# Zeroing the scratch tensors of an attention + MLP + expert kernel from SBUF instead of from a DRAM constant

## The reference, cut to what matters

```python
# 1. attention in a window of 128 with a linear bias, 8 heads of 64 channels
scores = scale * q @ k.T + bias, masked;  attn = softmax(scores);  x = attn @ v
# 2. a dense MLP, 512 -> 2048 -> 512
r = np.maximum(x @ w_in, 0.0);  x = (s * (r * r) + b) @ w_out
# 3. experts: each token goes to the best 2 of 8, with noisy logits
noisy_logits = x @ w_gate + np.log1p(np.exp(x @ w_noise)) * noise
top2 = np.argpartition(-noisy_logits, 2, axis=1)[:, :2]     # weights: softmax over the two
for e in range(8):
    for k in range(2):
        mask = top2[:, k] == e
        h = np.maximum(x[mask] @ w1[e], 0.0)                 # 512 -> 1024
        out[mask] += top2_w[mask, k, None] * (h @ w2[e])     # 1024 -> 512
```

## Time and profile before

| what | value |
|---|---|
| median of 3 runs | 1090.13 us (1089.6 to 1093.48) |
| the profiled execution's own time | 1090.13 us |
| its span in the profile | 1088.3 us |
| PE busy | 1044.8 us, 96% |
| DVE, ACT, POOL busy | 60%, 44%, 11% |
| mean granted TensorE clock | 0.987 of full speed |
| bytes moved by DMA | 147.04 MB, mean 135 GB/s |

### The profile page before, as it was taken

How to read it: one execution, slowest core, us unless ns; L and a number is a source line. 1 busy time by engine, 2 the same in 40 slices (tenths; PEclk the granted TensorE clock), 3 DMA queues, 4 the chain that set the end, 5 groups by cost and what they waited for, 6 DMA issues and landing times.

```text
span 1088.3 us, 18159 instructions
## 1 busy us (share of the span) xinstructions
PE 1044.8 (96%) x5846; PEld 917.1 (84%) x5847; DVE 656.6 (60%) x1955; ACT 479.1 (44%) x988; POOL 117.9 (11%) x122
## 2 busy tenths in 40 slices
PE   5689999999999999999999999999999999999995
PEld 4588889889889888988989888888888889888884
DVE  6777866766776686664567845654545435445322
ACT  6756665555556456443445333333323323233211
POOL 0000000110020020010020111211121111211211
PEclk9799999999999999999999999999999999999998
DMA  6556754454463343122364525352523515423312
GB/s 185 151 176 202 229 160 153 160 175 145 155 214 102 93 146 98 49 72 104 97 223 155 178 79 175 96 185 72 172 90 112 180 61 185 137 83 101 129 30 97
DMA packets 76473, 147.04 MB, mean 135 GB/s; under 512 B 12012, under 2 KB 12652, under 8 KB 76272
## 3 DMA queue, kind: packets, MB, share of 16 engines
q1 hardware_dynamic: 67440, 125.91, 36.8%
q0 software_dynamic: 8960, 20.21, 5.3%
HBM read 125.09 MB, written 46.78 MB: 158 GB/s over the span
## 4 chain that ended last, share of the span: by engine, by line
PE 89%; DVE 4%; ACT 3%; issue 2%; DMA 1%; SPq 0%; DVEq 0%; POOL 0%; ACTq 0%; POOLq 0%
PE bank L1300 23%; PE bank L1302 23%; PE bank L1301 23%; PE bank L1441 8%; PE bank L1281 3%; PE bank L1268 2%; PE bank L1326 1%; PE bank L1247 1%; PE bank L1449 1%; PE bank L1248 1%; PE bank L1387 1%; PE bank L1394 1%; DVE x_sc L837 1%; ACT x_sc L610 1%; ACT w_now_hi L664 1%
## 5 line engine op out<-in xcount | busy, mean ns | idle before, releaser
L1300 PE MATMUL bank<-w_hi,g_hi 128*128 128x512 f32 x312 | 127.5, 409 | 1.2 <-DVE g_lo L1182 1.2
L1302 PE MATMUL bank<-w_hi,g_lo 128*128 128x512 f32 x312 | 122.4, 392 | 0.0
L670 ACT ACTIVATE relu<-bank 128x384 f32<-128x384 f32 x96 | 47.1, 491 | 170.7 <-PE bank L1302 170.5
L1301 PE MATMUL bank<-w_lo,g_hi 128*128 128x512 f32 x312 | 121.9, 391 | 0.0
L892 DVE SCALAR_TENSOR_TENSOR relu<-relu,sb_scale 128x384 f32<-128x384 f32 x96 | 59.3, 618 | 70.5 <-ACT relu L670 70.5
L532 POOL DMA_INDIRECT rows_scratch<-x,slot x36 | 39.2, 1090 | 522.6 <-DVE x L973 513.4
L759 ACT ACTIVATE g_hi<-bank 128x384 fp32r<-128x384 f32 x56 | 27.5, 492 | 141.4 <-PE bank L1302 141.4
L610 ACT ACTIVATE x_sc<-x_sc,least 128x256 f32<-128x256 f32 (+1 forms) x144 | 69.9, 488 | 12.2 <-DVE least L837 11.9
L1149 DVE SCALAR_TENSOR_TENSOR g_lo<-bank,g_hi 128x384 fp32r<-128x384 f32 x56 | 31.1, 556 | 72.6 <-ACT g_hi L759 72.4
L886 DVE TENSOR_TENSOR w_now_lo<-stage_a,w_now_hi 128x1024 fp32r<-128x1024 f32 x48 | 58.7, 1223 | 23.0 <-ACT w_now_hi L664 22.8
L837 DVE CUSTOM_DVE_ANT_0 x_sc<-bank,nbias 128x256 f32<-128x256 f32 (+1 forms) x144 | 52.9, 405 | 30.9 <-PE bank L1248 22.5
(11 more groups left out here) (210 smaller groups left out, 2751.1 us busy)
## 6 DMA issues: line engine op xcount, KB each, us to landing
stage_a<-in_w_first SPq DMA_DIRECT2D x92, 256.0 KB, 2.9
stage_a<-in_w_second SPq DMA_DIRECT2D x92, 256.0 KB, 3.1
qk_raw<-in_qk SPq DMA_DIRECT2D x144, 128.0 KB, 2.7
y_scratch<-in_blank SPq DMA_DIRECT2D x13, 768.0 KB, 5.9
stage_b<-in_w_first SPq DMA_DIRECT2D x28, 256.0 KB, 2.9
stage_b<-in_w_second SPq DMA_DIRECT2D x28, 256.0 KB, 3.8
rows_scratch<-in_blank SPq DMA_DIRECT2D x8, 774.0 KB, 6.5
rows<-rows_scratch SPq DMA_DIRECT2D x8, 774.0 KB, 7.1
```

The lines of the kernel that those rows point to most:

```text
L670: act.activation(relu[:, (t * C1 + c) % GR, :], h_bank[c % 2][:, 0:TOK1], ACT.Relu).then_inc(relu_ready, 1)
L1300: pe.matmul(psum, lh, rh, start=(first and n == 0), stop=False)
L1301: pe.matmul(psum, lh, rl, start=False, stop=False)
L1302: done = pe.matmul(psum, ll, rh, start=False, stop=(last and n == len(pairs) - 1))
```

## The change

The constant `blank` is gone. In the head POOL clears the tile `x2` once (128 partitions x 1548 floats), then puts 2^20 in the last column of the tile's first block (`zeroed`). SP waits for that after the head, and then fills both scratch tensors from `x2`, all of it in stage 0. `rows_dram` takes 24 DMAs of 128 rows (258 KB each), three in each of the slots 2 to 9. `y_dram` takes 13 DMAs of 384 rows (768 KB each), one in each of the slots 2 to 14. Since the first `copy_out` overwrites `x2`, ACT and DVE wait there until all 37 have landed (`zero_out`). The waits for `rows_blank` on POOL and `y_blank` on SP go.

```diff
+        zeroed = sem("zeroed")
+        zero_out = sem("zero_out")
+        ZEROS = (E * BLK2 + YROWS // TOK2) * 16
...
+                sp.wait_ge(zeroed, 1)
...
-                        if t == 0 and c % 2 and 3 <= c < 3 + 2 * E:
-                            at_ = (c - 3) // 2 * N
-                            sp.dma_start(rows_dram[at_:at_ + TOK2, :], a["blank"]).then_inc(rows_blank, 16)
-                        if 1 <= t and c % 2 and 3 <= c < 15:
-                            r = ((t - 1) * 6 + (c - 3) // 2) * TOK2
-                            if r < YROWS:
-                                sp.dma_start(y_dram[r:r + TOK2, :], a["blank"][:, 0:DM]).then_inc(y_blank, 16)
+                        if t == 0 and 2 <= c < 2 + E:
+                            for r in range(BLK2):
+                                at_ = (c - 2) * N + r * P
+                                sp.dma_start(rows_dram[at_:at_ + P, :], x2[:, 0, :]).then_inc(zero_out, 16)
+                        if t == 0 and c >= 2:
+                            for r in range((c - 2) * TOK2, min((c - 1) * TOK2, YROWS), TOK2):
+                                sp.dma_start(y_dram[r:r + TOK2, :].rearrange("(p b) d -> p b d", b=BLK2),
+                                             x2[:, :, 0:DM]).then_inc(zero_out, 16)
...
-                    sp.wait_ge(y_blank, YROWS // TOK2 * 16)
...
                 pool.tensor_copy(seam[:], seam_f).then_inc(seam_cast, 1)
+                pool.memset(x2[:], 0.0).then_inc(cleared, 1)
+                pool.wait_ge(cleared, 1)
+                pool.memset(x2[:, 0, DM + 3:RW], NOWHERE).then_inc(zeroed, 1)
                 pool.memset(ones[:], 1.0).then_inc(const_done, 1)
...
-                pool.wait_ge(rows_blank, E * 16)
...
+                    act.wait_ge(zero_out, ZEROS)
                     act.activation(x2[:, 0, 0:DM], out1[0][:], ACT.Copy).then_inc(x2_copied, 1)
...
+                    dve.wait_ge(zero_out, ZEROS)
                     for j in (1, 2):
                         dve.tensor_copy(x2[:, j, 0:DM], out1[j][:]).then_inc(x2_copied, 1)
```

More of the change, by code:

```diff
@@ L240, in build @@
         nbias_cast = sem("nbias_cast")
+        cleared = sem("cleared")
         const_done = sem("const_done")
@@ L257, in build @@
         w_ready = sem("w_ready")
-        rows_blank = sem("rows_blank")
-        y_blank = sem("y_blank")
+        zeroed = sem("zeroed")
+        zero_out = sem("zero_out")
         h_ready = sem("h_ready")
@@ L1541, in constants @@
     seam[0, 3 * P:3 * P + P // 2] = -8.0 * NEG
-    blank = np.zeros((TOK2, RW), np.float32)
-    blank[:, DM + 3] = NOWHERE
     return {
-        "blank": blank,
         "ident": np.eye(P, dtype=np.float32),
```

## The result

The changed kernel takes 1104.64 us (median of 4 runs, 1101.93 to 1105.37) beside 1091.11 us (4 runs) for the kernel before: the medians are 13.5 us apart. The ratio, which goes by more runs than these (seven of the changed kernel), is 1.0113, 95% interval 1.0089 to 1.0138, which is 12.3 us. The forecast was 1093.1 us, range 1089.3 to 1099.0. Its direction holds, and so does the backlog that it named; the size does not, nor does the road by which the backlog reaches PE, and the time lies outside the range. Two more series of the same kernel gave 1.0087 and 1.0098, so 8 to 14 us are lost, never 3.

A forecast was written before the change was run, and what follows sets the result against it. The prediction took PE, busy 96% of the span, as the bound. Its terms, 0 + 2.7 + 0 + 0.3 = +3.0 us on 1090.13 us, gave 1093.1 us, range 1089.3 to 1099.0.

The forecast's parts named there:

- Part 1: Stages 1 to 3: the 13 old copies leave, hidden by PE's own work; gain 0, bounds 0 to 1.0 us.
- Rival C: Stages 1 to 3, calmer, give back at most 1.0 us, nothing lost in stage 0: 1089.1 us; chance 0.03.
- Part 2: Stage 0's DMA queue: 15.0 MB ahead of slot 10's weights make them 4.6 us late; 2.7 us reach PE.
- The rate: Stage 0's queue: 63% stores at 375 and 37% at 331 GB/s give 357 GB/s; 15.0 MB take 42.0 us.
- rival B: Stage 0: writes slower in a long queue; 1096.8 us at 331 GB/s, 1100.2 us at 314; chance 0.20.
- The start: Slot 4's load, issued by 86.2 us, finds the queue about empty; the sum of bytes starts there.
- The absorption: Behind slot 10's late weight conversion, 1.9 of 4.6 us are absorbed before PE's next scores; 2.7 us reach PE.
- The bias road: Stage 0: DVE's `add_bias` queues behind the late conversion and PE's scores wait for it; 2.7 us reach PE.
- Stand in it, and do not pass: Stage 0: weight rounds wait behind the fills on SP's queue; a store behind one landed after 4.8 us, others 3.6.
- Part 3: First `copy_out`: fills landed at 147.1 us, copies due at 148.1, so the new wait costs nothing.
- Part 4: Head: POOL's memset blocks a DVE instruction, 0.3 us taken, between 0 and 1.7; SP's extra issues cost nothing.
- Rival D: Stage 0: PE's new waits bring one clock drop, 1.8 us on top of 3.0: 1094.9 us; chance 0.04.

The follow-up runs named there:

- memsets only: The kernel before with POOL's two memsets of `x2` in the head and nothing else of the change: 1090.60 us.
- the two repeats: The changed kernel, unedited, measured in two more series, each beside the kernel before: 1098.48 us and 1099.03 us.
- one more tensor: The changed kernel with one more DRAM tensor of 2.3 MB, of which only 8 KB are written: 1100.65 us.
- the two kernels with long pieces: The changed kernel with each slot's three row fills as one DMA of 6192-byte pieces, 1097.30 us; the same with y fills of 6144-byte pieces too, 1097.67 us.
- three more fills: The changed kernel plus three fills of 768 KB behind slots 4, 6 and 8, into a tensor nobody reads: 1103.41 us.
- all eleven late runs of the table: Table of the changed kernel and its variants; late ones had slot 10's weight rounding later than the kernel before, by up to 12.6 us.
- fills on POOL's queue: The changed kernel with all 37 fills issued by POOL instead of SP, each slot's once its weights are converted: 1107.07 us.
- all in long pieces: The changed kernel with row fills in 6192-byte pieces and y fills in 6144-byte pieces from a second zero tile: 1097.67 us.

## Why the prediction failed in size

**Part 1, gain 0: right** within the 0 to 1.0 us it allowed. From the copies into `x2` to the end the changed kernel is at most 0.6 us shorter. The span behind them goes by half-clock stretches: 942.9 us before, 942.6 with memsets only (which keeps the old copies) and 942.6, 942.3 in the two repeats, with one stretch each; 944.1 to 945.6 in four kernels with two; 945.8 to 946.7 in five with three, the changed one among them. Rival C is out.

**Part 2, the backlog: right in kind, 7.6 us too small at PE** (forecast 2.7, measured 10.3). Three terms were mis-sized. They add up by construction, since the second is what the others leave over:
- The rate. 357 GB/s was a mix of short stretches. The full queue ran at 327 in this execution: 15.0 MB take 45.9 us instead of 42.0, +3.9. This is rival B's idea, and at its 331.
- The start. "With the queue about empty" at 86.2 us was wrong: the share is full from 74 us on (1.04 from 74 to 86 us), and the weight load issued at 84.5 us landed after 4.6 us instead of 3.0. What is left over when 86.2 (moved by each kernel's head) + bytes / rate + 1.3 is set against the measured rounding is 1.9 us here, and 1.8 to 3.3 us in the repeats, with one more tensor, in the two kernels with long pieces and with three more fills. +1.9. It fits what was moved: from 84.5 to 132.3 us it was 329 GB/s, 15.7 MB, some 0.7 MB or 2 us more than the 15.0 MB of the sum. Lateness 4.6 + 3.9 + 1.9 = 10.4, as measured.
- The absorption. "1.9 us are absorbed" was the step that failed outright. I followed DVE's bias to PE's scores, and by the rows of a beat ahead of the rounding. Behind slot 10's rounding the copy of `pT` comes first: it stands in ACT's own queue, and PE's value product waits for it with 0.1 us of slack. In all eleven late runs of the table PE lost, up to that product, what slot 10 was late, less 0.1 us. +1.8. The bias road exists as well, one slot earlier and not absorbed either: 3.03 us of PE's wait in the profiled execution.

With all their fills in stage 0 the kernels' queues had, for 34 us, 327 to 369 GB/s with 2-KB pieces and 381 to 383 with pieces of 6 KB in some or all fills. By the limit of about 358 GB/s per core that the Trainium skill gives (DMA: Bandwidth & Descriptors, Specifications) the sum had come out at my value. The rates lie on both sides of it and all under the 435 of the same section; the measurement decides. What I had counted as agreement of rows and limit was a coincidence of short stretches.

**The mechanism itself is shown, not argued:** spreading the same fills removes the loss, taking away the y fills or thinning either kind removes most of it or all, more bytes add to the lateness, and a faster rate for the same bytes lessens it. What sets the rate of a full queue is not shown. "Stand in it, and do not pass" was half the truth: a queue of its own did not protect the weights. With the DMA share at 1.05 it is the 16 engines' time that is short; what a better place in the line alone would give, no run tells.

**Part 3, costs nothing: right** in the changed kernel, though not by its own dates: the last fill was issued at 150.26 us, not 139.2, since SP was late as well, and PE was later still. The fills on POOL's queue show the other side of it.

**Part 4: the sign of the mechanism right, the size not to be seen.** The blocked instruction was `total_eps`, not `k_lo`, and lost 1.2 us, not 0.44. The rows have 1.33 us for it beside one memset and 2.90 beside two. The Trainium skill (SBUF — State Buffer, SBUF: two separate sides) names two kinds of DVE instruction that a GpSimd instruction can block: one with two SBUF inputs, only against a GpSimd instruction that reads SBUF, and one in a 2-port perf mode, without that condition. The forecast named the first kind alone; `total_eps` has one input, so only the second kind could cover it, and no trace here shows an instruction's mode. In the time of the kernel no loss was measured.

**Rival D, the clock: underrated at 0.04.** All runs in which PE was held up by over 2 us in stage 0 but one (all in long pieces) have one or more half-clock stretches between 107 and 144 us, and none of the four without a long wait has. That such stretches follow PE's waits is what I take from it; no run switched them alone. One of 3.4 us that falls on a busy PE costs about 1.5 us: from the value product to the copies it is 17.2 us in the kernels with one there and 15.6 or 15.7 in those without. Of the profiled execution's 14.1 us all but the queue's 10.3 are of this kind (-1.67 + 2.44 + 3.06 = 3.8). In another execution they fall otherwise, which is the spread between the series. Adding rivals B and D, instead of setting them against each other, would have given 1096.8 + 1.8 = 1098.6 us, the level of the two repeats, but partly by luck: both kept the 1.9 us of absorption.

## What to carry to other kernels

Before work is moved into a stage, sum its bytes against a queue that is *full*, from the moment it fills and at the lowest rate that any mixed stretch shows, and spread what can't be late evenly over all that is in time. When a conversion will be late, go through every instruction queued behind it on its own engine and ask who waits for each; the first one without slack is what counts, and only then the others. Moving low-priority transfers to another queue did not shield the urgent ones here: spacing them did, and fewer DMAs with longer pieces helped in part.

## What the runs showed of the hardware

- A full queue of stores and loads moved 327, 342, 343 and 353 GB/s with pieces of 2048 and 2064 bytes in the three executions of the changed kernel and the one with one more tensor, 369 with three more fills of 768 KB, and 381, 383 with pieces of 6 KB in the rows' fills and in all fills. The 353 and the 369 came without any change in the pieces' length.
- With the fills on POOL's queue, weight loads on SP's queue still landed after up to 10.2 us, where the earlier trace rows has 2.9.
- SP's issues themselves grew with the backlog; its timeline at 100 us, where three issues take 3.31 us (the shortest of the kind takes 0.43):
```profile
99.54 0.43 SPq L344 DMA_DIRECT2D stage_a<-in_w_second  x1
100.02 3.31 SPq L441 DMA_DIRECT2D rows_scratch<-x  x3
103.37 0.67 SPq L444 DMA_DIRECT2D y_scratch<-x  x1
```
- A memset on POOL of 128 x 1548 held up a DVE instruction of two elements a row from its start to its end.
- Executions of one kernel differ by up to 6 us (the kernel before: 1086.77 to 1092.85 on one chip), and in the profiled ones the time behind the first stage goes with the count of 3.4-us stretches at half clock in it: 942.3 to 942.9 us with one, 945.8 to 946.7 with three.
